# Two FFN layers of matrix products as seven block products of a 2x2 split instead of eight

## What is computed

```python
for c in range(nc):                       # 24 chunks of 32 queries, context 56 keys + 8 memory keys
    scores = scale * np.matmul(q_c, k_full.transpose(0, 1, 3, 2))
    ...
    out[:, :, c_start:c_end] = np.matmul(a, v_full)
...
def _moe_ref(x, w_in, w_out):
    h = x @ w_in
    g = np.where(h > 0.0, h, alpha * (np.exp(np.minimum(h, 0.0)) - 1.0))
    return (g @ w_out).astype(np.float32)
...
def _moe2_ref(x, w_in, w_out, s, b):
    h = x @ w_in
    r = np.maximum(h, 0.0)
    g = s * (r * r) + b
    return (g @ w_out).astype(np.float32)
```

## Time and profile before

| what | us |
|---|---|
| median of 3 runs | 1239.18 (1238.47 to 1241.78) |
| span of the profiled execution | 1237.6 |
| TensorE matmul busy | 1218.2 (98%) |
| VectorE busy | 663.4 (54%) |
| ScalarE busy | 432.2 (35%) |
| GpSimd busy | 163.0 (13%) |
| first FFN matmul starts | 43.12 |

### The profile page before, as it was taken

The page is one execution under the profiler, slowest core; times in us unless marked ns, Lnnn a source line. Parts: engine busy times, 40 slices in busy tenths (PEclk is TensorE's granted clock), DMA queues, the critical chain, the costliest instruction groups (busy, mean ns, idle before and its releaser), DMA issues.

```text
span 1237.6 us, 21026 instructions
## 1 busy us (share of the span) xinstructions
PE 1218.2 (98%) x7336; PEld 1129.5 (91%) x7336; DVE 663.4 (54%) x1721; ACT 432.2 (35%) x1217; POOL 163.0 (13%) x135
## 2 busy tenths in 40 slices
PE   8899999999999999999999899999999999999998
PEld 5688999999999999999999899999999999999997
DVE  7887555656555556465656754344343434343433
ACT  4434443434444434343432223222222323232322
POOL 3796000000000000000049920000000000000000
PEclk8999999999999999999999899999999999999999
DMA  6653121212112112212023301001010101010000
GB/s 118 151 138 88 49 47 32 63 39 54 32 38 57 37 31 64 47 49 59 6 86 102 128 26 52 0 2 48 0 51 0 51 0 51 0 51 0 25 0 25
DMA packets 124046, 58.62 MB, mean 47 GB/s; under 512 B 92280, under 2 KB 116856, under 8 KB 124024
## 3 DMA queue, kind: packets, MB, share of 16 engines
q1 hardware_dynamic: 119800, 52.05, 17.1%
q10 hardware_dynamic: 4224, 6.29, 1.4%
HBM read 45.75 MB, written 12.58 MB: 47 GB/s over the span
## 4 chain that ended last, share of the span: by engine, by line
PE 94%; DVE 4%; issue 1%; ACT 0%; DMA 0%; SPq 0%; DVEq 0%
PE bank L429 43%; PE bank L447 42%; PE bank L381 3%; PE bank L403 2%; PE bank L390 2%; PE bank L367 1%; PE bank L356 1%; DVE bank L616 1%; DVE P L629 1%; DVE x_lo L647 1%; DVE act_e L656 0%; DVE rowsum L625 0%; DMA k_nat<-in_mem_k 0%; DVE g_lo L669 0%; DVE rowmax L616 0%
## 5 line engine op out<-in xcount | busy, mean ns | idle before, releaser
L429 PE MATMUL bank<-x_hi,wu_hi 128*128 128x384 f32 x1024 | 353.4, 345 | 4.4 <-DVE x_lo L647 4.3
L429 PE MATMUL bank<-x_hi,wu_lo 128*128 128x384 f32 x1024 | 346.0, 338 | 0.0
L429 PE MATMUL bank<-x_lo,wu_hi 128*128 128x384 f32 x1024 | 345.4, 337 | 0.0
L537 ACT ACTIVATE act_e<-bank 128x384 f32<-128x384 f32 x256 | 125.4, 490 | 389.4 <-PE bank L429 389.3
L544 ACT ACTIVATE g_hi<-g_raw 128x384 fp32r<-128x384 f32 x256 | 134.8, 526 | 273.1 <-DVE g_raw L664 156.9
L669 DVE TENSOR_TENSOR g_lo<-g_raw,g_hi 128x384 fp32r<-128x384 f32 x256 | 157.8, 616 | 97.9 <-ACT g_hi L544 97.8
L429 PEld LDWEIGHTS bank<-x_hi,wu_hi 128*128 128x128 f32 x1024 | 193.8, 189 | 13.0 <-DVE x_lo L647 5.1
L429 PEld LDWEIGHTS bank<-x_lo,wu_hi 128*128 128x128 f32 x1024 | 194.0, 189 | 4.7
L429 PEld LDWEIGHTS bank<-x_hi,wu_lo 128*128 128x128 f32 x1024 | 193.4, 189 | 0.0
L662 DVE TENSOR_TENSOR act_e<-act_e 128x384 f32<-128x384 f32 x128 | 76.0, 594 | 212.5 <-ACT act_e L537 212.5
L447 PE MATMUL bank<-g_hi,wd_hi 128*128 128x384 f32 x512 | 178.5, 349 | 0.3 <-DVE g_lo L669 0.3
(11 more groups left out here) (65 smaller groups left out, 1182.2 us busy)
## 6 DMA issues: line engine op xcount, KB each, us to landing
w_raw<-in_moe_w_in SPq DMA_DIRECT2D x32, 256.0 KB, 2.8
w_raw<-in_moe_w_out SPq DMA_DIRECT2D x32, 256.0 KB, 3.1
x_scratch<-y_sb ACTq DMA_DIRECT2D x8, 768.0 KB, 3.8
x_raw<-x_scratch SPq DMA_DIRECT2D x8, 768.0 KB, 5.4
q_nat<-in_q SPq DMA_DIRECT2D x30, 192.0 KB
v_nat<-in_v SPq DMA_DIRECT2D x23, 240.0 KB
out<-y_sb SPq DMA_DIRECT2D x7, 768.0 KB, 4.0
k_nat<-in_k SPq DMA_DIRECT2D x22, 240.0 KB
```

The costliest lines, as they stand in the source:

```text
L429: last = nc.tensor.matmul(pH[f % 2][:, 0:TOK], wu[:, kk, w], x[:, kk, :], start=(kk == 0 and i == 0), stop=(kk == KT - 1 and i == 2))
L537: nc.scalar.activation(act_e[:, f % 2, :], pH[f % 2][:, 0:TOK], (ACT.Exp, ACT.Relu)[layer]).then_inc(e_done, 1)
```

## The change

Each layer is computed in tiles of 1024 tokens: 3 tiles a layer, 6 in all (`t`). A tile has two groups (`gr`), each over half of the 2048 inner features, and a group has an up phase and a down phase of 28 steps each. A step (`step_at(g)`, 672 of them) is 6 matmuls of 128x512 into one or two PSUM banks. In a phase, operands are taken as 2x2 blocks and the product as seven block products P1 to P7, in the order P1, P6, P2, P7, P5, P4, P3, so that 7 x 6 matmuls stand where eight products would need 8 x 6.

- **Sums of the right operand.** For x, four sums a half (GpSimd `sums_of_x`, VectorE `sums_head` for the first tile); for g, `sums_t1_t2`, `sum_t3`, `sum_t4` on VectorE, 16 of 128x512 a down phase. Seven blocks are cut into hi and lo instead of four.
- **Sums of the products.** The results are put together from `s1`, `s2`, `s3` (`copy_s1` on ScalarE, `combine`, `add_y`, `add_y11` on VectorE).
- **Nonlinearity.** For layer 0 two ScalarE passes and one VectorE pass (`relu_of`, `exp_of`, `elu_of`), for layer 1 `relu_h11`, `square_of`, `affine`.
- **Weights.** GpSimd makes seven blocks of each set of 2x2 weight blocks (`prepare`: 4 sums and 7 cuts, each over 128x256), 16 sets a layer. Each product's block (hi and lo, 256 KB) is saved by an SP transfer to `w_scratch` from a ring of 3 (`save_weights`), and every step reads its own back: 512 KB for two steps (`load_weights`), a ring of 4.
- **Attention.** 11 units run ahead of the FFN with two input buffers; the other 21 are woven in, one every 7 steps, 11 into tile 0 and 10 into tile 1.
- **Output.** The result of layer 1 stands transposed, so 24 blocks of four transposes, a ScalarE copy and a store follow (`transpose_out`, `copy_out`, `save_out`).
- The program has no loops left; the instructions of all steps are written out.

```diff
+HALF = 512
+TOK = 2 * HALF
...
+HEAD = 11
+WEAVE = 7
+WOVEN = [(HEAD + c, WEAVE * c) for c in range(11)] + [(HEAD + 11 + c, PER_TILE + WEAVE * c) for c in range(10)]
...
+SPLIT_AT = (90, 100)
...
+            def load_v(n):
+                b, blk = divmod(n, UPB)
+                if n >= 2:
+                    sp.wait_ge(pv_done, n - 1)
...
+            for n in range(HEAD):
+                load_qk(n + 2)
+                for _ in range(3):
+                    save_weights(saves)
+                    saves += 1
+                load_v(n + 2)
+                if n >= 5 and n - 5 < W_RING:
+                    load_weights(n - 5)
...
+                if d < PER_TILE // 2:
+                    due = min(PRODUCTS, 33 + 2 * (d - W_RING + 1))
...
+            def transpose_p(n, e):
+                at = banks_of(n)
+                pe.wait_ge(P_ready, 2 * n + e + 1)
+                if n < HEAD:
+                    if e == 0 and n:
+                        pe.wait_ge(PT_sb[0], n)
+                    if e == 1:
+                        pe.wait_ge(kT_sb, min(n + 3, HEAD))
...
+            def down(st):
+                k = split_of(st)
+                pe.wait_ge(g_lo_done, k + 1)
...
+            for n in range(HEAD + 1):
+                if n < HEAD:
+                    score(n)
+                if n + 1 < HEAD:
+                    transpose_k(n + 1)
+                    transpose_q(n + 1)
+                idle_products(3)
+                if n:
+                    transpose_p(n - 1, 0)
+                    transpose_p(n - 1, 1)
+                    idle_products(2)
+                    p_times_v(n - 1)
...
+                if t < TILES:
+                    if 0 <= s < 4:
+                        sums_t1_t2(t, gr, s)
+                    if 7 <= s < 11:
+                        sum_t3(t, gr, s - 7)
+                    if 15 <= s < 19:
+                        sum_t4(t, gr, s - 15)
...
+                if g + 2 < STEPS and not step_at(g + 2).up:
+                    lo_g(step_at(g + 2))
+                for xt, kk, i in x_split_at(g - 1):
+                    lo_x(xt, kk, i)
```

More of the change, by code:

```diff
@@ new lines, with layer, round, phase @@
+@dataclass
+class Step:
+    t: int
+    gr: int
+    up: bool
+    u: int
+    pi: int
+    i: int
+    g: int
+    @property
+    def layer(self):
+        return self.t // TPL
+    @property
+    def round(self):
+        return 6 * self.t + 3 * self.gr + (self.u if self.up else 2)
+    @property
+    def phase(self):
+        return 2 * self.t + self.gr
+    @property
+    def j(self):
+        return 2 * self.u + self.i if self.up else self.i
+def step_at(g):
+    t, s = divmod(g, PER_TILE)
+    gr, s = divmod(s, GROUP)
+    if s < PHASE:
+        return Step(t, gr, True, s // 14, s % 14 // 2, s % 2, g)
+    return Step(t, gr, False, 0, (s - PHASE) // QUADS, s % QUADS, g)
@@ L305, in _ @@
+            for g in range(STEPS - 8, STEPS + 1):
+                for ot, tb in out_block_at(g):
+                    save_out(ot, tb)
+            for i in range(2):
+                sp.wait_ge(out_saved[i], 16 * (TPL * OUT_BLOCKS // 2))
         @block.gpsimd
@@ new lines, in add_y, with elu_of @@
+            def add_y(st, s, made, b):
+                for d in range(2):
+                    dve.wait_ge(made, 2 * st.round + d + 1)
+                    nc.vector.tensor_tensor(s[:, d, :], s[:, d, :], y_at(b, d), ALU.add).then_inc(y_sums, 1)
+            def elu_of(st):
+                m = item_at(st)
+                dve.wait_ge(exp_of_h, m + 1)
+                g = X[:, {P2: X11, P5: X22, P4: X21, P3: X12}[st.pi], st.j, :]
+                h = acc_a[st.i][:, :] if st.pi == P2 else g
+                nc.vector.scalar_tensor_tensor(out=g, in0=elu[:, m % 4, :], scalar=-1.0, in1=h, op0=ALU.add,
+                                               op1=ALU.max).then_inc(elu_done, 1)
@@ L742, in _ @@
[L742 to L753 removed]
+                    copy_PT(n - 1)
```

1226 lines of the change are left out of this document (777 added, 449 removed).

## The result

The changed kernel takes 1444.61 us (median of 4 runs, 1440.32 to 1449.78), the kernel before 1240.48 beside it: a ratio of 1.164, interval 1.1592 to 1.1687. The forecast was 1376 (a ratio of 1.110), with a range up to 1470. Direction and range hold; the slowdown is 16.4% instead of 11%, and the 63 us between a forecast span of 1375 and the measured 1437.9 have to be found.

What follows compares the result with a forecast made beforehand. TensorE's matmuls were taken to bound the kernel before. Head 190, TensorE's FFN work 1027, phase changes 42, x cut 40, x load 5, GpSimd 60 and end 11 gave a span of 1375, so 1376 us; range 1235 to 1470.

Steps and rivals of the forecast that it cites:

- head to the first FFN matmul: Attention units ahead of the FFN: first FFN matmul at 190 us instead of 43.12, with rounds of load plus chain, 16.5 each.
- columns: 672 steps: TensorE in the FFN: 2,064,384 columns at 0.4534 ns take 936.0 us, against 1069.8 before.
- change of phase, group 0: Where up turns to down: VectorE's bunched operations make g_lo late, TensorE stalls 3.5 us in each of 12 phases, +42.
- cut of x: Group 1 down phases: 56 VectorE operations outlast 19 TensorE steps, stalling about 8 us in each of 5 tiles, +40.
- woven units: Attention units woven into the FFN: 21 instead of 28, at the earlier 3.80 us each, 79.8 us.
- GpSimd beside VectorE: Tiles 0 to 2: GpSimd's weight cutting slows VectorE's operations with two SBUF inputs, +37, +15 and +8, together +60 us.
- the signs that the prediction named: In the profile after: first FFN matmul near 190, k_nat gaps of 5 us or more, g_lo stalls, VectorE over 90% busy.
- The first rival: In the FFN: TensorE goes on setting the pace, with VectorE operations under 0.47 us; 1230, or 1195 with shorter head; 15%.
- The second rival: In the head: the load is off the loop, a round is the chain alone, 9.9 us; 1323; 13%.
- The third: In tile 0: weights set the pace if contention stretches a product to 3 us; +60 to +100, 1460; 12%.
- ScalarE has at most 44 operations: Down phases that cut x: ScalarE's operations take 26 us, so ScalarE is no bound.
- The prediction's term for ScalarE's waits: Where x is cut: ScalarE's wait for the 1 MB load of x may add 0 to 20 us; 5 taken.

Runs made afterwards that it cites:

- e4_both_small: Changed kernel with VectorE's lo parts of the next tile's x and GpSimd's sums of x both cut to 8 columns: 1379.00 us.
- e10_all_three: Changed kernel with head q and k loaded ahead of v, and x lo parts, GpSimd's x sums and its weight work on 8 columns: 1281.34 us.
- e5_small_w: Changed kernel with GpSimd's sums and cuts of weight blocks on 8 of 128 columns, transfers and waits kept: 1390.66 us.
- e1_head_order: Changed kernel with q and k of unit n+3 loaded ahead of v of unit n+2 in the head's SP order: 1404.50 us.
- e6_extra_ops: Changed kernel with four unused VectorE operations of 96x512 added to each down phase of layer 1: 1460.13 us.
- e3_small_x_sums: Changed kernel with GpSimd's eight sums of x a tile cut from 512 to 8 columns, waits kept: 1402.70 us.
- e12_score_order: On top of e1_head_order, a unit's 16 score products alternate between even and odd heads: 1395.37 us.

## Why the prediction was right in direction and too small

By its own steps, forecast and measured, in us. Where a row names no run, the number is of the changed kernel.

| step | forecast | measured | difference |
|---|---|---|---|
| head to the first FFN matmul | 190 | 184 | -6 |
| columns: 672 steps | 936 | 672 x 38.1 / 28 = 914 | -22 |
| change of phase, group 0 | 6 x 3.5 | 6 x 4.8 | +8 |
| the same, group 1, without the cut | 6 x 3.5 | 6 x 8.8, with 2 transposed blocks | +32 |
| cut of x | 5 x 8, + 5 for loads | 63 (`e4_both_small` against changed, five phases) | +18 |
| woven units | 21 x 3.80 = 80 | 68 + 54 = 122 (`e10_all_three`) | +42 |
| GpSimd beside VectorE | 60 | 49 (`e5_small_w`) | -11 |
| output transposes in the FFN | 11 | 2 x 3.8 (41.9 - 38.1), and 2 blocks above | -3 |
| waits for `w_ring` at the start of tiles 2 and 3 | 0 | 4.8 + 1.5 (42.9 and 39.6 less 38.1) | +6 |
| end | 11 | 10 | -1 |

The differences sum to +63, all that is missing. That they close so well is luck in part: the rows come from four runs, and a phase of tiles 0 to 2 differs by 1 to 3 us from run to run. The range held in part by luck too. The sum's own upper bound, 1450, held by 5 us, and only because 22 us too much for columns, 11 for GpSimd and 6 for the head stood against what was missing.

Of the signs that the prediction named, the first FFN matmul, the spacing of the rounds, the lower clock and the stalls for `g_lo` came. TensorE's gaps on `k_nat` are 4.0 us in the mean and not 5 or more, since it works on scores beside the load. Tiles 2, 3 and 4, with 197.5, 180.8 and 183.3, lie above the 165 to 180 that it gave; tile 5 lies inside. In the down phase of tile 3 above VectorE is 85% busy, not over 90%.

**The head was right in mechanism and size.** The load of 6.4 (6.6), the chain of 9.5 (9.9), the eight rounds and the lower clock are as told, and `e1_head_order` took the load out of the loop. I expected 45 to 55 for that and got 40: a round without the load is 10.7 and not 9.9, since the prediction's chain left out the scores, which only the load had hidden.

**The first rival fell.** It wanted VectorE's operation at 0.47 or less. It costs 0.60 in a row (1057.62 to 1058.22 above, and `e6_extra_ops`), next to the 0.61 of the forecast. The second rival, load off the loop, fell with the k transposes that DMA released. The third, weights that pace tile 0, is half true: GpSimd and its saves stand on the chain there, and saving 44 more blocks ahead shortened the tile by 12. Waits for `w_ring` cost 6 us more in tiles 2 and 3. But its price of 60 to 100 did not come, since `e5_small_w`, which takes nearly all of GpSimd's work away, shortened tile 0 by 20.

**Columns were too dear by 2.3%.** The 0.4534 ns came from a mix of 384 and 512 columns. A phase of 512 alone runs at 38.1 / (28 x 3072), 0.443 ns.

**The step that failed first: the stall at a change of phase, 3.5 in each of 12.** The mechanism was right (`e6_extra_ops`) and the size was not: 4.8 in group 0. TensorE's seven steps last 9.5 us and not 9.75, which is 0.2 of the 1.3 too little, the two short pauses are 0.4, and the rest stays open. In group 1 the prediction counted the VectorE operations right but let only the change of phase stall, and 8.8 were measured. In tile 5, with no cut of x, three more gaps stand further on (0.58, 0.69 and 0.80 in the records, 2.8 us by their starts), behind the `add_y` pairs.

**The step that failed second: the cut of x was priced on VectorE alone.** "ScalarE has at most 44 operations [...] no bound" was true of its work and false of its waits. The diff and the order had `sums_of_x` on GpSimd, ahead of `xc_hi` on ScalarE, and the prediction named GpSimd beside VectorE only for the weights. `e3_small_x_sums` gives 42 us to these eight operations a tile. The prediction's term for ScalarE's waits, "0 to 20; I take 5", was for the load of x alone, and what that load costs TensorE was not isolated. A second term stood at nothing, the clock in the FFN. Behind these stalls TensorE ran at the lower level, which cost 15 us in the five phases and 2 in those of `e4_both_small`.

**The step that failed third: a woven unit keeps the 3.80 of before.** That price was read where TensorE never idled. Here a unit costs 5.8. Of the surplus of 2.0, some 1.5 are idle time (`e10_all_three`) and 0.5 is the order of the score products, but giving the 0.5 back shortened tiles 0 and 1 by 3 us only (`e12_score_order`). In the changed kernel TensorE idles between 184 and 450 us for P (13.3), for copies of PT (4.2 and 3.4) and for k (2.4), though also 11.2 for `g_lo`. So I take the idle time to be the attention chain's, which a unit must run through in 7 steps. That is read from waits and not shown by an experiment, and stays open; so does what part the saves have, which stand on the SP queue ahead of the units' loads.

**GpSimd beside VectorE** was near in sum (60 against 49) but spread wrongly: 37, 15 and 8 forecast for tiles 0 to 2, against 20, 14 and 14. In tile 0 the woven units cover part of it; in tile 2 the down phase of group 0 alone lost 14 (57.8 to 43.6 in `e5_small_w`).

## What to carry to other kernels

Removing an eighth of the matmuls pays only if the additions that replace them fit under what is left: count operations by engine for each phase, not for the kernel, and find the 7 steps in which they bunch. Follow each value through all engines that it passes and take the waits with it, GpSimd's too, even if that engine is mostly idle. And when code is written anew, check that loads stand ahead of waits they don't need, and that small matmuls keep their order.
